# Chunked linear attention woven into two feed-forward layers: factors made two slots ahead, row copies issued late by one queue

## What is computed

```
for t in range(S):                       # q, k, v, a: 4 batches x 8 heads x 768 steps x 48
    new_re = ar * S_re - ai * S_im       # a is scaled by min(|a|, 0.999) / (|a| + 1e-6)
    new_im = ar * S_im + ai * S_re
    S_re, S_im = new_re + outer(k[t], v[t]), new_im
    y[t] = q[t] @ S_re                   # S is 48 x 48 for each batch and head
x = y as (3072 tokens, 384)
h = x @ w_in;  x2 = (h * clip(h + 3, 0, 6) / 6) @ w_out           # 384 -> 2048 -> 384
h = x2 @ w2_in; out = (max(h, 0) + alpha * min(h, 0)) @ w2_out    # 384 -> 2048 -> 384
```

## Time and profile before

| | |
|---|---|
| median of the runs shown | 1109.07 us |
| the profiled execution: its own time | 1106.7 us |
| its span, first to last instruction | 1105.0 us |
| mean granted TensorE clock | 0.953 |
| TensorE busy | 975.5 us (88%) |
| VectorE busy | 684.8 us (62%) |
| ScalarE busy | 486.3 us (44%) |
| GpSimd busy | 315.3 us (29%) |

### The profile page before, as it was taken

How to read it: one execution, slowest core, us unless ns; L and a number is a source line. 1 busy time by engine, 2 the same in 40 slices (tenths; PEclk the granted TensorE clock), 3 DMA queues, 4 the chain that set the end, 5 groups by cost and what they waited for, 6 DMA issues and landing times.

```text
span 1105.0 us, 16686 instructions
## 1 busy us (share of the span) xinstructions
PE 975.5 (88%) x6178; PEld 957.3 (87%) x6178; DVE 684.8 (62%) x1210; ACT 486.3 (44%) x814; POOL 315.3 (29%) x291
## 2 busy tenths in 40 slices
PE   0456676998998998979989999999999999999998
PEld 0456666998998998979989999999999999999998
DVE  7756888787887897987888425453434343443432
ACT  5536655565665766566655335332212121122211
POOL 0234331222222221222222233333333333333332
PEclk9858798899998999999999999999999999999999
DMA  8551232333232332323322170101011010101000
GB/s 170 140 148 33 66 94 75 87 85 91 81 78 68 91 86 75 95 74 89 98 63 76 41 261 14 43 2 43 1 44 40 5 44 1 44 1 43 1 23 23
DMA packets 84803, 72.84 MB, mean 66 GB/s; under 512 B 34928, under 2 KB 80496, under 8 KB 84336
## 3 DMA queue, kind: packets, MB, share of 16 engines
q1 hardware_dynamic: 75120, 63.43, 21.0%
q10 hardware_dynamic: 9600, 8.33, 2.9%
HBM read 40.90 MB, written 9.44 MB: 46 GB/s over the span
## 4 chain that ended last, share of the span: by engine, by line
PE 54%; DVE 19%; issue 8%; SPq 8%; ACT 6%; DMA 3%; ACTq 1%; DVEq 0%
PE hp L1027 9%; PE hp L1029 8%; PE hp L1028 8%; PE op L1027 8%; PE op L1029 8%; PE op L1028 8%; SPq L358 4%; DVE gated L775 3%; DVE t_inv L676 2%; SPq L350 2%; DVE prod L740 2%; DVE t_fb L706 2%; DVE t_fb L734 2%; PE gp L990 2%; DMA st<-prod 2%
## 5 line engine op out<-in xcount | busy, mean ns | idle before, releaser
L465 POOL TENSOR_TENSOR g_lo<-gated,g_hi 128x384 fp32r<-128x384 f32 x256 | 280.6, 1096 | 705.2 <-ACT g_hi L554 705.2
L554 ACT ACTIVATE g_hi<-gated 128x384 fp32r<-128x384 f32 x256 | 133.6, 522 | 338.3 <-DVE gated L789 290.1
L785 DVE TENSOR_SCALAR gate<-hp,alpha_sb 128x384 f32<-128x384 f32 x128 | 79.1, 618 | 229.3 <-PE hp L1029 229.3
L1027 PE MATMUL hp<-x_parts,wa_hi 128*128 128x384 f32 x384 | 136.0, 354 | 33.7 <-DMA x_parts<-x_parts 33.7
L775 DVE SCALAR_TENSOR_TENSOR gated<-gate,hp 128x384 f32<-128x384 f32 x128 | 69.4, 542 | 134.7 <-ACT gate L547 134.6
L1027 PE MATMUL op<-g_hi,wb_hi 128*128 128x384 f32 x384 | 135.6, 353 | 0.3 <-ACT out_sb L559 0.3
L1029 PE MATMUL hp<-x_parts,wa_lo 128*128 128x384 f32 x384 | 132.0, 344 | 0.0
L1028 PE MATMUL hp<-x_parts,wa_hi 128*128 128x384 f32 x384 | 131.9, 343 | 0.0
L1029 PE MATMUL op<-g_hi,wb_lo 128*128 128x384 f32 x384 | 130.5, 340 | 0.0
L1028 PE MATMUL op<-g_lo,wb_hi 128*128 128x384 f32 x384 | 130.5, 340 | 0.0
L1027 PE MATMUL op<-g_hi,wa_hi 128*128 128x384 f32 x384 | 129.9, 338 | 0.0
(11 more groups left out here) (96 smaller groups left out, 1858.3 us busy)
## 6 DMA issues: line engine op xcount, KB each, us to landing
st<-prod SPq DMA_DIRECT2D x48, 145.1 KB, 3.1
st<-prod ACTq DMA_DIRECT2D x48, 145.1 KB, 2.8
a_sb<-a_in SPq DMA_DIRECT2D x24, 288.0 KB, 3.4
qk_sb<-qk_in SPq DMA_DIRECT2D x24, 288.0 KB, 3.5
v_pad<-v_in SPq DMA_DIRECT2D x24, 192.0 KB, 3.3
x<-out_sb SPq DMA_DIRECT2D x8, 576.0 KB, 3.0
x_raw<-x SPq DMA_DIRECT2D x8, 576.0 KB, 4.6
out<-out_sb SPq DMA_DIRECT2D x8, 576.0 KB, 3.1
```

What stands on the lines that cost most here:

```text
L465: pool.tensor_tensor(g_lo[:, at, :], gated[:, at * UT:(at + 1) * UT], g_hi[:, at, :].bitcast(F32), ALU.subtract).then_inc(glo_done, 1)
L554: act.activation(g_hi[:, at, :], gated[:, at * UT:(at + 1) * UT], ACT.Copy).then_inc(ghi_done, 1)
L785: dve.tensor_scalar(gate[:, at], hp[:, n % 2, 0:UT], 0.0, alpha_sb[:, m:m + 1], ALU.min, ALU.mult).then_inc(gate_done, 1)
L1027: pe.matmul(acc, lhs[0], rhs[0], start=start, stop=False)
```

## The change

The three quantities of a slot come from three functions of their own, and the attention has one slot more:

```diff
-FIRST_SLOT = -3
+FIRST_SLOT, LAST_SLOT = -3, NCH + 1
-W_SPLITS = {0: 5, 1: 5, 2: 5, 3: 4, 4: 5}
-ITEMS = {CPU: 3, CPU + 1: 4, CPU + 2: 3, CPU + 3: 4}
+W_SPLITS = {0: 4, 1: 4, 2: 4, 3: 4, 4: 4, 5: 4}
+ITEMS = {CPU + 1: 4, CPU + 2: 3, CPU + 3: 3, CPU + 4: 3}
+def scores_at(s):
+    c = s - 1 if s <= CPU else s - 2
+    return c if 0 <= c < NCH and s != CPU + 1 else None
+def factors_at(s):
+    c = s + 1 if s < CPU - 1 else s
+    return c if 0 <= c < NCH and s != CPU - 1 else None
+def decays_at(s):
+    c = s + 2 if s < CPU - 2 else s + 1
+    return c if 0 <= c < NCH and s != CPU - 2 else None
```

SyncE's queue and ScalarE's:

```diff
@@ sync
-                sp.wait_ge(prod_done, 2 * c + 2)
-                for to, rows in high_stack(c, 1, HIGH_PARTS[:2]):
-                    sp.dma_start(to, rows).then_inc(st_landed[c % 2], 16)
+                if c >= CPU:
+                    sp.wait_ge(prod_done, 2 * c + 2)
+                    for to, rows in low_stack(c, 1) + high_stack(c, 1):
+                        sp.dma_start(to, rows).then_inc(st_landed[c % 2], 16)
...
-                if pos == 2:
-                    if c1 is not None:
+                if pos == 3:
+                    if c1 is not None and c1 < CPU:
                         stack(c1)
                     if c0 is not None:
                         spread(c0)
+                    if c1 is not None and c1 + 1 < NCH:
+                        load_qk(c1 + 1)
+                    if c0 is not None and c0 + 1 < NCH:
+                        load_v(c0 + 1)
+                    if c1 is not None and c1 >= CPU:
+                        stack(c1)
+                    if c2 is not None and c2 + 2 < NCH:
+                        load_a(c2 + 2)
...
@@ scalar
             def stack(c):
+                need(act, y_ready, c - 1)
+                need(act, state_ready, kept(c - 1))
                 act.wait_ge(prod_done, 2 * c + 2)
-                for to, rows in low_stack(c, 1) + high_stack(c, 1, HIGH_PARTS[2:]):
+                for to, rows in low_stack(c, 1) + high_stack(c, 1):
                     act.dma_start(to, rows).then_inc(st_landed[c % 2], 16)
...
-                if pos == 1 and c1 is not None:
+                if pos == 1 and c2 is not None:
+                    magnitude(c2)
+                if pos == 2 and c1 is not None:
                     waves(c1)
-                if pos == 2 and c0 is not None:
+                if pos == 3 and c0 is not None:
                     x_high(c0)
                 if n is not None:
                     high(n + GSTEP)
...
-                if pos == 2 and c2 is not None:
-                    magnitude(c2)
-                if pos == 3 and c1 is not None:
+                if pos == 3 and c1 is not None and c1 < CPU:
                     stack(c1)
```

More of the change, by code:

```diff
@@ L71, in w2o_tiles @@
     return [k for k in ((2, 3) if m == 0 else (m + 3,)) if k < MT_FF]
[L74 to L82, removed]
+def scores_at(s):
[7 more added lines that the diff above has]
+    return c if 0 <= c < NCH and s != CPU - 2 else None
 def items_through(s):
-    if s <= CPU + 3:
+    if s <= CPU + 4:
         return sum(count for t, count in ITEMS.items() if t <= s)
-    return sum(ITEMS.values()) + (s - CPU - 3) * MT_FF // CPU
+    return sum(ITEMS.values()) + (s - CPU - 4) * MT_FF // CPU
 def items_of(s):
@@ L101, in places @@
 def places():
-    for s in range(FIRST_SLOT, NCH + 1):
+    for s in range(FIRST_SLOT, LAST_SLOT + 1):
         items = items_of(s)
         for pos in range(max(POSITIONS, len(items))):
-            yield (s, pos, items[pos] if pos < len(items) else None, chunk_at(s), chunk_at(s + 1), chunk_at(s + 2),
-                   chunk_at(s + 3))
-N_ATT = items_through(NCH)
+            yield (s, pos, items[pos] if pos < len(items) else None, scores_at(s), factors_at(s), decays_at(s),
+                   decays_at(s + 1))
+N_ATT = items_through(LAST_SLOT)
 def is_first(c):
@@ L271, in low_stack, with high_stack @@
                      prod[r * HD:(r + 1) * HD, x, :, :, :].rearrange("p k q t -> p k (q t)")) for r in range(2)]
-        def high_stack(c, x, parts):
+        def high_stack(c, x):
             return [(st[x * HD + d0:x * HD + d0 + rows, c % 2, h, :, :].rearrange("p q t -> p (q t)"),
-                     prod[p0:p0 + rows, x, k, :, :].rearrange("p q t -> p (q t)")) for p0, rows, k, h, d0 in parts]
+                     prod[p0:p0 + rows, x, k, :, :].rearrange("p q t -> p (q t)")) for p0, rows, k, h, d0 in HIGH_PARTS]
         def x_cols(c):
@@ L488, in _ @@
                     split_w(w)
-                if s == CPU - 1 and pos == POSITIONS - 1:
+                if s == CPU and pos == POSITIONS - 1:
                     for k in range(GSTEP):
@@ L824, in _ @@
                         forward(c1)
-                        phases(c1)
                 if pos == 1:
                     if c1 is not None:
+                        phases(c1)
                         fractions(c1)
@@ L833, in _ @@
                         mask(c0, 1)
+                if pos == 2:
                     if c1 is not None:
+                        if c1 == 0:
+                            dve.wait_ge(pads_set, 3)
                         backward(c1)
[L836 to L841, removed]
-                    if c0 is not None:
-                        x_low(c0)
+                        factors(c1)
                     if c2 is not None:
@@ L846, in _ @@
                         numerators(c2)
+                if pos == 3:
+                    if c1 is not None:
+                        products(c1)
+                    if c2 is not None:
                         inverse(c2, 0)
+                    if c0 is not None:
+                        x_low(c0)
                 if pos == 4:
-                    if c0 is not None and not is_last(c0):
-                        state(c0)
                     if c2 is not None:
@@ L854, in _ @@
                         ratios(c2)
-                if s == CPU - 1 and pos == POSITIONS - 1:
+                    if c0 is not None and not is_last(c0):
+                        state(c0)
+                if s == CPU and pos == POSITIONS - 1:
                     for k in range(GSTEP):
@@ L1091, in _ @@
                     second_half(n)
-                if s == CPU - 1 and pos == 3:
+                if s == CPU and pos == 4:
                     for k in range(HSTEP):
```

16 lines of the change are left out of this document (3 added, 13 removed).

## The result

| | before | after |
|---|---|---|
| median | 1108.87 us (7 runs, 1104.22 to 1110.28) | 1118.2 us (7 runs, 1115.57 to 1121.91) |
| the profiled execution: its own time | 1106.7 | 1117.12 |
| its span | 1105.0 | 1115.3 |
| granted TensorE clock, mean | 0.953 | 0.974 |

The ratio is 1.0097, with an interval of 1.0073 to 1.0121. I had forecast 1090.5 and a range of 1071 to 1108, and given "slower" a chance of 0.14. The wait that I expected to go has gone, the gates come when I said they would, and the kernel is still 28 us behind the forecast.

A forecast was written before the change was run, and what follows sets the result against it. It took TensorE to bound the kernel, with at most 6.4 of each 75.8 us (three slots) winnable and VectorE close behind. Gains 3 + 5 x 2.7 + 2 = 18.5 from 1106.7 gave 1088, 1090.5 as a median; range 1071 to 1108.

The forecast's parts named there:

- Part 1: TensorE's steady wait for `x_parts`: removed, since the spread goes ahead of the copies; gain 3.2 to 4.9 us per three slots.
- Part 2: TensorE's wait for `st` at a slot's start: removed, as the copies have one slot more; no separate size.
- Part 3: VectorE's later state makes five-item slots a ring of 24.05 us; net gain 2.7 us per three slots.
- Part 4: SyncE's ring with twelve copies on one queue: 15.3 us from `x_low` to `factors`, 0.35 to spare; put at nothing.
- rival (c): SyncE's ring binds through wider copy spacing: 26.9 us for every slot, 1129 us, slower; chance 0.1.
- Both rings: VectorE's slot through state and score, 24.05 us; SyncE's from `x_low` through copies to `factors` and back, 23.7 us.
- Part 5: ScalarE's reordering: nothing, slightly good; `waves` no longer holds back `high`, a gain already counted in VectorE's gate waits.
- Part 6: The start, with one slot without items added: net gain 3 us, uncertain by 8 either way.
- Part 7: The last slots, where VectorE lacks decays and factors, run at TensorE's pace: some 2 us won.
- Rival (a): State not binding, all TensorE waits go, 6.4 us per three slots: 37 us won, 1072; chance 0.2.
- (b): Rival: VectorE's `numerators` and `products` stretch beside GpSimd, ring 25.2 us, about 1106 for a median; chance 0.15.
- (d): Rival: the spread still arrives late, 3 to 5 us return per three slots, about 1108; chance 0.05.

The follow-up runs named there:

- a_xlow: The kernel after with `x_low(c0)` moved to the head of VectorE's position 3, nothing else; 1108.84 us, ratio 1.0006 to the kernel before.
- b_state_last: The kernel before with only `state(c0)` moved behind the two inverses and the ratios in VectorE's position 4; 1151.51 us, ratio 1.0387 to the kernel before.
- a_old_order: The kernel after with VectorE's and ScalarE's orders of the kernel before, keeping its two slots of lead and SyncE order; 1096.63 us, ratio 0.9899 to before.
- a_state_loads_xlow: The kernel after with `state` first in position 4, q, k, v loads ahead of the spread, and `x_low` first in position 3; 1063.41 us, ratio 0.9606 to before.
- a_state_xlow: The kernel after with `state` first in position 4 and `x_low` first in position 3; 1072.26 us, ratio 0.9658 to the kernel before.

## Why the prediction was wrong

**One slot read closely.** In the kernel after, the slot of chunk 8 (262.58 to 287.50) has six items: I had forecast 25.2 us for it, with the state ready at 24. TensorE's score, then VectorE:

```profile
262.58 1.13 PE L999 MATMUL gp<-st 96*128 96x128 f32 x8 [2.10 <-DVE s_pad L772]
...
267.85 0.55 DVE L782 SCALAR_TENSOR_TENSOR gated<-gate,hp 128x384 f32<-128x384 f32 x1 [1.78 <-ACT gate L556]
...
272.23 0.55 DVE L782 SCALAR_TENSOR_TENSOR gated<-gate,hp 128x384 f32<-128x384 f32 x1 [0.49 <-ACT gate L556]
...
274.79 0.17 DVE L735 COPY prod<-t_fb 128x6 f32<-128x6 f32 x1 [0.87 <-DMA st<-prod]
...
282.49 0.62 DVE L760 TENSOR_TENSOR x_parts<-yp,x_parts 128x512 fp32r<-128x512 f32 x1
...
286.80 0.56 DVE L772 TENSOR_TENSOR s_pad<-s_sum,st 96x384 f32<-96x384 f32 x1
```

And SyncE's queue over the same time:

```profile
258.22 3.81 SPq L356 DMA_DIRECT2D x_parts<-x_parts  x6
262.07 0.60 SPq L313 DMA_DIRECT2D qk_sb<-qk_in  x1
...
263.88 0.60 SPq L331 DMA_DIRECT2D v_pad<-v_in  x1
264.59 5.04 SPq L364 DMA_DIRECT2D st<-prod  x6
...
269.67 3.85 SPq L368 DMA_DIRECT2D st<-prod  x6
```

The gates of positions 1 and 2 stand at 5.27 and 9.65 us in the slot, with waits of 1.78 and 0.49; I had said 5.3 and 9.7, with 1.6 and 0.75. The copy into `prod` waits 0.87 us for the last of the twelve copies, where I had it pass with 0.35 to spare. The state ends at 287.36, 24.8 us into the slot, and the next score starts 0.14 us later: VectorE's round is 24.9 us, the forecast 24.05 and the wait of 0.87. TensorE is done with its six items at that same moment, so this slot takes 24.92 and shows no wait at its end. From the end of `x_low`, ahead of the spread at 258.2, to the copy into `prod` 16.6 us go by, not 15.3. The first six copies took 5.04 us instead of 3.87: one of the six issues took 1.81 us, the others 0.59 to 0.60. So SyncE's ring is 16.6 + 8.3 = 24.9. The slot behind it (chunk 9) has five items and the forecast of 24.05. In it, it is the landing that is late. Its twelve issues went out at the usual pace and ended at 297.27, and the copy into `prod` started 3.1 us later, against 1.3 in the slot above; from `x_low`'s end at 283.11 it is 17.3 us:

```profile
289.50 3.88 SPq L364 DMA_DIRECT2D st<-prod  x6
293.42 3.85 SPq L368 DMA_DIRECT2D st<-prod  x6
...
300.39 1.02 DVE L735 COPY prod<-t_fb 128x6 f32<-128x6 f32 x1 [1.54 <-DMA st<-prod]
...
313.49 1.99 PE L999 MATMUL gp<-st 96*128 96x128 f32 x8 [4.11 <-DVE s_pad L772]
```

That slot takes 25.99 us, and here TensorE waits: 4.11 us, where I had said about 2. The eight five-item slots of the twelve take 23.93 to 26.61, 25.15 in the mean. The four with six items take 22.76 to 24.86, 24.2 in the mean and less than the 25.2 forecast: two of them are the last chunk of a batch, without a new state, in which TensorE has some 156 matmuls instead of 181.

**What a wait does to the slot behind it.** Two scores of the kernel after, and the five us of TensorE's work behind each (columns of a window: start and end, its length, busy us and count of PE, PEld, DVE, ACT and POOL, granted clock, DMA share, GB/s):

```profile
386.45 2.05 PE L999 MATMUL gp<-st 96*128 96x128 f32 x8 [3.73 <-DVE s_pad L767]
...
413.06 1.13 PE L999 MATMUL gp<-st 96*128 96x128 f32 x8 [2.10 <-DVE s_pad L772]
```

```profile
386.45:391.50 5.05, 5.05 (x20) 5.05 (x21) 3.43 (x10) 1.40 (x3) 1.78 (x1) 0.50 0.68 154
413.06:418.10 5.04, 5.04 (x36) 5.04 (x37) 3.45 (x10) 1.39 (x3) 1.52 (x1) 1.00 0.82 172
```

Behind the wait of 3.73 us the granted clock was 0.50 (1.2 GHz) and TensorE did 20 matmuls in the five us; behind the wait of 2.10 it was 1.00 (2.4 GHz) and it did 36. The five-item slot from 386.45 took 26.61 us, the longest of the twelve. So such a wait is paid twice: at the lower clock `hidden` ends later, and VectorE gets the gate of position 1 after a wait of 4.45 us, 7.9 us into the slot instead of 5.3, with no wait for the copies in that slot:

```profile
394.36 0.56 DVE L782 SCALAR_TENSOR_TENSOR gated<-gate,hp 128x384 f32<-128x384 f32 x1 [4.45 <-ACT gate L556]
```

The three five-item slots of the twelve whose score stood behind waits of 3.73 to 4.11 us had a mean granted clock of 0.89 to 0.93 and took 25.5 to 26.6 us; four of the other five, at 0.98 to 1.00, took 23.9 to 24.7, and the fifth is the 25.99 above. But the length of the wait doesn't decide it. In a_xlow a score behind a wait of 2.09 us had 0.50, and in b_state_last one behind 3.63 us had 0.66:

```profile
551.22:556.30 5.08, 5.08 (x20) 5.08 (x21) 3.43 (x10) 1.02 (x2) 1.50 (x1) 0.50 0.46 108
...
476.75:481.80 5.05, 5.04 (x25) 5.05 (x26) 4.59 (x13) 1.51 (x4) 1.34 (x1) 0.66 0.64 170
```

**Point by point.**

- *Part 1, the wait for x_parts:* right. None in the steady slots of the kernel after (two waits in all, both in the start).
- *Part 2, the wait for st:* right.
- *Part 3, the state later:* the mechanism was right and its size was not. The gates came as said and the state ends the slot. But 24.05 us was 25.15 in the mean of the five-item slots, and up to 26.6 where the clock fell, which has no term in my sum. Forecast gain in twelve slots 10.8 us, measured 5.3.
- *Part 4, SyncE's ring, "I put it at nothing":* mis-sized. 15.3 us was 16.6 and 17.3, with the spare 0.35 turned into waits of 0.87 and 1.54. The bound that I kept for it, in rival (c), was a wider spacing in every slot; what came was a single long issue in one slot and a late landing in the next. Both rings were in my text. What I didn't say is that each feeds the other: `x_low`, `products` and the state are behind the copy that waits.
- *Part 5, ScalarE, "nothing, slightly good":* no run has the change without this part alone, so its worth isn't measured; a_old_order points to more than nothing. Besides the waits for fractions, ScalarE loads the tables of its functions (`ACT_TABLE_LOAD`) 48 times for the 24 chunks where it did so 72 times, at 1.28 us each. That is its 31 us of less work, and it has no term in my prediction.
- *Part 6, the start, "net gain 3 us, uncertain by 8":* this is the step of the prediction that failed, with 23.8 of the 28.8 us. The timeline of the kernel after, before its steady slots:

```profile
75.44 0.61 SPq L331 DMA_DIRECT2D v_pad<-v_in  x1
...
109.05 0.69 PE L1036 MATMUL hp<-x_parts,wa_hi 128*128 128x384 f32 x1 [9.10 <-DMA x_parts<-x_parts]
...
127.78 1.05 PE L999 MATMUL gp<-st 96*128 96x128 f32 x8
162.65 2.05 PE L999 MATMUL gp<-st 96*128 96x128 f32 x8 [9.49 <-DVE s_pad L772]
186.82 2.05 PE L999 MATMUL gp<-st 96*128 96x128 f32 x8 [6.63 <-DVE s_pad L772]
...
211.76 0.69 PE L1036 MATMUL hp<-x_parts,wa_hi 128*128 128x384 f32 x1 [6.77 <-DMA x_parts<-x_parts]
```

  I had 68 for the load of v (75.44), 99 for the first `hidden` (109.05), 120 for chunk 3's score (127.78), 146 and 169 for the next two (162.65 and 186.82), and 194 for item 13's `hidden` (211.76). The load of v stood behind the spread, which I had counted for the later chunks and not here, and each later row bears the lateness of the one before. Of the 23.8 us that were missed up to chunk 9, 17.8 are there at item 13, and 6 came in the next three slots. My two criteria for "wrong" in part 6, the first `hidden` beyond 107 and chunk 3 not before 128, come out met and missed by 0.2 us.

  The runs show what the loss is made of. The empty slot and the depth don't make it by themselves: a_state_loads_xlow has both and starts chunk 9 at 265.56. It is the late order on VectorE together with SyncE's queue: the state moved forward brings that score from 287.50 to 283.12, the loads alone to 284.26, both to 272.24. By my own terms for the start and the first three slots that score was due at 272.50 - 5.7 - 3.1 = 263.7. With the two rings out of the way the forecast for the start holds to 2 us, but by luck in part, since its steps don't hold: the same kernel has chunk 4's score at 154.96 and chunk 5's at 176.29, behind waits of 6.77 and 3.90 us, and makes it good in the later slots. How much of those two waits is the slots' own VectorE work, I haven't separated.
- *Part 7, the end:* right, 2 forecast and 2.5 left over in the ledger.

**The rivals.** Rival (c) had the right mechanism, the right sign and 1129, with a place (all slots) and a cause (spacing) that were not the ones found; it was worth more than 0.1. Rival (a), all waits gone, is what a_state_loads_xlow does: I gave 1072, and it gave 1063.41. It could go below (a) because the 6.4 us per three slots that I took for all there was to win were reckoned from TensorE's busy time at the clock of before, 69.45 us; without the waits the clock stays at 1.00 and the same work takes 66.56. Of (b) a little is there: VectorE is busy for 255.27 us in the twelve slots instead of 250.96, 0.36 us a slot. In the slot above the first operation of `numerators`, the one of the earlier trace rows, takes 0.55 us again (at 277.26), but `clip` just before it takes 1.37. It isn't what decides: a_state_xlow has 253.64 and no wait left. Nothing speaks for (d): the spread is never waited for in the steady slots.

## What to carry to other kernels

Where several engines run through one loop in step, write down each ring (who waits for whom, round to the next slot) and its length, and treat two rings within one or two us of each other as binding: put a term for it in the sum, and shorten both before judging either, since here one alone won 8 or 15 us and the two 44. In an in-order queue, put first what another engine waits for (state, `x_low`, the loads of the next chunk), and only then the work that has a slot of time; here the deeper lead made the kernel faster than the one before only where the state came first. And when TensorE is made to wait, look at the granted clock behind the wait before pricing it at the wait's own length.

## What was not expected of the hardware

- A wait of 3.73 us at the score was followed by a granted clock of 0.50, and the eight score matmuls took 2.05 us in place of 1.13; one of 2.10 us was not, and one of 2.09 in a_xlow was. b_state_last has such scores too; how much of its 43 us they are wasn't measured apart.
- Among SyncE's issues of 0.59 to 0.65 us single ones took 1.8 us, and the same copies landed 1.3 us after their last issue in one slot and 3.1 in the next. What they wait for, the trace doesn't say. In a plan with 0.35 us to spare either is enough.
